# Rounding the mixed output weights in four pieces instead of two, in a fused attention and two-layer kernel

## The chip, the cores and the metric

The kernel runs on one core of one Trainium2 chip. The metric is the time of one execution on the device in microseconds (us), as the median of several runs. The core has five engines that run side by side and meet through semaphores: PE (matmuls, with its weight loads as PEld), DVE (VectorE), ACT (ScalarE), POOL (GpSimd) and SP, which here only issues DMAs.

## What is computed

```python
scores = scale * np.matmul(q, k.transpose(0, 1, 3, 2))        # 4 x 8 heads, 576 tokens, head size 64
thresh = np.max(scores, axis=-1, keepdims=True) - tau
scores = np.where(scores >= thresh, scores, -1000000000.0)
attn = softmax(scores)                                         # written out in the reference
x = np.matmul(attn, v)                                         # as 2304 x 512
h = x @ w_in                                                   # 512 x 2048
g = h * np.tanh(log1p(exp(h)))
x = g @ w_out                                                  # 2048 x 512
h = x @ w_in2
x = (h * np.clip(h + 3.0, 0.0, 6.0) / 6.0) @ w_out2
```

## The kernel before

The program has two stages. The first, some 330 us, is attention. The second, some 715 us, is the two layers, whose products are done by a scheme of seven products for eight (Strassen's, in Winograd's form), so each block of weights is needed as seven "mixes": sums and differences of its quarters. Each operand is split in a high part (the value rounded to the PE's fast 32-bit format, fp32r) and a low part (the rest), and three products of parts stand for one.

**Attention** walks over 32 heads in 8 turns (`it`) of 4 heads. A turn has 18 steps (`s`): two pairs of heads with 9 tiles of queries each, so steps 0 to 8 and 9 to 17 are two alike halves. In step `s`, by `attention_step` of each engine:

- PE makes the scores of tile t in two halves of 288 columns (L548), then spreads the sums in the third and fourth steps of a half (L581) or multiplies by the values (L601) in the other steps, then transposes tile t-2: first its tail of columns (L556), then the four main squares (L560). Before the second half of the scores it waits until ACT has kept the tail of tile t-2 (`after(pe, tail_kept, t - 2)`, with t that of the next step), and before the main squares until ACT has kept the main part of the tile before.
- ACT copies the transposed tail out of PSUM (`keep_tail`, L774), makes the exponentials of tile t (L793), and copies the transposed main part (`keep_main`, L758). In the third and fourth steps of a half a copy of the spread sums (L786) stands ahead of the tail. After steps 3 and 5 it rounds a head's keys (`round_k`, L745).
- DVE takes the maximum (L1010), weighs tile t-1 (L994), makes the threshold (L1021), and in steps 0 and 9 adds a small number to nine sums (`totals`, L1026) and inverts them. In steps 1, 6, 10 and 15 it scales an output (L1001); PE's spreading of sums waits for those of steps 1 and 10.
- POOL splits queries and keys of the coming heads (L1271 to L1283). In its order of one turn stand also, in this place: split of head 0, `mix_prep_in`, `mix_prep_out`, split of head 1, split of head 2, `rest_prep`, split of head 3. The split of head 2 ends with a wait for ACT's `round_k` of step 3.

**Preparation of the output weights.** A unit is one of 8 slices of one layer's output weights: 7 mixes of 256 columns on 128 partitions. It goes through `prep_out` (loaded by SP, mixed by POOL at L1300 or DVE at L1143), `prep_high` (rounded by ACT, `round_prep`, L806) and `prep_low` (`prep_out` less `prep_high`: `rest_prep`, POOL at L1306 for the first seven units, DVE at L1149 for the other nine), and SP stores both to DRAM (`store_prep_high`, `store_prep_low`). `PREP_PARTS` says in which pieces L806 and the subtractions are done:

```python
PREP_PARTS = (slice(0, 4), slice(4, MIXES))
...
if s == 16 and it < ITS - 1:
    round_prep(0, it, 0)
if s == 1 and it > 0:
    round_prep(0, it - 1, 1)
```

So seven units are rounded within the attention, one a turn: four mixes (1024 columns) after the `keep_main` of step 16, three (768 columns) after that of step 1 of the next turn. POOL's `rest_prep` of the unit comes after its wait for step 3. The other nine units are prepared in the layers (`late_unit`, `late_part`), in groups of products whose order on each engine is fixed in the code.

The order on every engine is that of the program; nothing reorders it. A wait holds all that stands behind it on its engine.

Of the kernel before, what the change touches and what calls it, by code (L numbers as in the profile page):

```python
# [14 lines left out]
def after(engine, semaphore, count):  # L15

    if isinstance(count, int) and count <= 0:
        return
    engine.wait_ge(semaphore, count)


def attention_and_layers(nc, qT, kT, v, tau, w_in1, w_out1, w_in2, w_out2, out):
# [16 lines left out]
    ITS = HEADS // HEADS_IT  # L39
# [13 lines left out]
    MIXES = 7  # L53
    A11_B11, S1_T1, S2_T2, S3_T3, A12_B21, S4_B22, A22_T4 = range(MIXES)
    QUADS = DFF // (2 * P)
# [96 lines left out]
    with ExitStack() as ctx:  # L152
# [3 lines left out]
        def sem(name):  # L156
            return ctx.enter_context(nc.semaphore(name))
# [51 lines left out]
        prep_out_rounded = sem("prep_out_rounded")  # L209
        prep_out_split = sem("prep_out_split")  # L210
# [37 lines left out]
        def f32(ap):  # L248
            return ap.bitcast(F32)

        def head_used(it, k):


            return it * TILES_IT + PAIR_TILES * (k // 2) + (MAIN + 1, PAIR_TILES)[k % 2]
# [47 lines left out]
        def late_unit(n):  # L302
            return divmod(QUADS - 1 + n, QUADS)


        def late_part(r, q):
            return divmod(GROUPS * r + q, 3) if r < SPANS else (LATE_UNITS, q)


        PREP_PARTS = (slice(0, 4), slice(4, MIXES))  # L310

        def g_slot(t, s):
            return t[:, s % G_RING, :]
# [47 lines left out]
        def _(sp):  # L361
# [44 lines left out]

            def store_prep_high(layer, u):

                sp.wait_ge(prep_out_rounded, 2 * (QUADS * layer + u) + 2)
                dst = w_out_mix[layer][:, u, :, :].rearrange("m p (h n) -> p m h n", h=2)  # L410
                sp.dma_start(dst[:, :, 0, :], f32(prep_high[:, :, :])).then_inc(prep_out_stored, 16)

            def store_prep_low(layer, u):

                sp.wait_ge(prep_out_split, 2 * (QUADS * layer + u) + 2)
                dst = w_out_mix[layer][:, u, :, :].rearrange("m p (h n) -> p m h n", h=2)
                sp.dma_start(dst[:, :, 1, :], f32(prep_low[:, :, :])).then_inc(prep_out_stored, 16)

# [49 lines left out]
            for r in range(ROUNDS):  # L468
                for q in range(QUADS):
                    unit, part = late_part(r, q)  # L470
# [265 lines left out]
        def _(act):  # L736
# [42 lines left out]
            def attention_step(it, s, ahead=True):  # L779

                t, p, i = it * TILES_IT + s, s // PAIR_TILES, s % PAIR_TILES
                first = isinstance(it, int) and it == 0
                if i in (2, 3) and (not first or p == 1):
                    u, pair = i - 2, it * PAIRS_IT + p - 1
                    act.wait_ge(spread_ready, 2 * pair + u + 1)
                    nc.scalar.copy(spread[:, PART_AT[u]:PART_AT[u + 1]], mixed[u]).then_inc(spread_kept, 1)  # L786
                if (not first or s >= 2) and (ahead or s < 2):
                    keep_tail(t - 2, (s - 2) % TILES_IT, it * PAIRS_IT + (s - 2) // PAIR_TILES)
                if ahead:
                    act.wait_ge(max_ready, t + 1)  # L790

                    after(act, probs_ready, t - 1)
                    nc.scalar.activation(halves(exps[:, s % 2, :]), scores[s % 3], ACT.Exp,  # L793
                                         bias=neg_max[:, s % 3:s % 3 + 1], scale=1.0).then_inc(exp_ready, 1)
                if (not first or s >= 2) and (ahead or s < 2):
                    keep_main(t - 2, (s - 2) % TILES_IT)
                if ahead and s in rounds:
                    round_k(it, rounds[s])

            def round_prep(layer, u, half):  # L800

                unit = QUADS * layer + u
                act.wait_ge(prep_out_mixed, 4 * unit + 4)
                after(act, prep_out_stored, 32 * unit)
                mixes = PREP_PARTS[half]
                nc.scalar.copy(prep_high[:, mixes, :], prep_out[:, mixes, :]).then_inc(prep_out_rounded, 1)  # L806

            def round_x(r, m):

                if m in X_MIXES:  # L810
                    act.wait_ge(x_mixed, 4 * r + X_MIXES.index(m) + 1)
                elif 0 < r < SPANS:
                    act.wait_ge(x_ready, 2 * PAIRS)
                elif r == 0:
                    act.wait_ge(x_ready, 4 * PAIRS_BATCH)
                else:
                    act.wait_ge(blocks_added, adds_before(r - SPANS + 1, 0))
                    act.wait_ge(c11_kept, r - SPANS + 1)
                after(act, slot_used, slots_before(r - 1, True))
                plain = {A11_B11: B11, A12_B21: B21, S4_B22: B22}  # L820
                src = x_block(r, plain[m]) if m in plain else x_mix[:, m, :, :]
                nc.scalar.copy(x_high[:, m, :, :], src).then_inc(x_high_ready, 1)
# [66 lines left out]
            for it in range(ITS):  # L889
                for s in range(TILES_IT):  # L890
                    attention_step(it, s)
                    if s == 16 and it < ITS - 1:
                        round_prep(0, it, 0)
                    if s == 1 and it > 0:
                        round_prep(0, it - 1, 1)
                    if it == ITS - 2 and s in (8, 10, 12):
                        round_x(0, X_ORDER[(8, 10, 12).index(s)])
                    if it == ITS - 1 and s in (2, 4, 6, 8):
                        round_x(0, X_ORDER[3 + (2, 4, 6, 8).index(s)])
                    if it == ITS - 1 and s == 16:  # L900
                        act.wait_ge(k_low_ready[HEADS_IT - 1], ITS)
                        act.wait_ge(scores_ready, head_used(ITS - 1, 1))
                        round_w(0, 0, 0)
                    if it == ITS - 1 and s == 17:
                        round_w(0, 0, 1)
# [15 lines left out]
            for r in range(ROUNDS):  # L921
                for q in range(QUADS):
                    if (r, q) == (0, 0):
                        continue
                    keep_first(r, q)
                    if q + 1 < QUADS:
                        round_w(r, q + 1, 0)
                    else:
                        for s in range(3):
                            round_g(r, s)  # L930
                    if q > 0:
                        gate(r, q - 1, B21)
                    if q + 1 < QUADS:
                        round_w(r, q + 1, 1)
                    else:
                        for s in range(3, G_RING):
                            round_g(r, s)
                    unit, part = late_part(r, q)
                    if unit < LATE_UNITS and part == 1:
                        for half in range(2):  # L940
                            round_prep(*late_unit(unit), half)
                    for b in (B22, B11, B12):
                        gate(r, q, b)
                gate(r, QUADS - 1, B21)
                for s in range(G_RING, SLOTS):
                    round_g(r, s)
                    if s == 13:
                        keep_first(r, QUADS)
                    if s == 45:
                        keep_c11(r)  # L950
                    if r + 1 < ROUNDS and s in ROUND_X_AT:
                        round_x(r + 1, X_ORDER[ROUND_X_AT.index(s)])
                if r + 1 < ROUNDS:
                    round_w(r + 1, 0, 0)
                    round_w(r + 1, 0, 1)
# [3 lines left out]
        def _(dve):  # L959
# [184 lines left out]

            def rest_prep(layer, u):

                for half, mixes in enumerate(PREP_PARTS):
                    dve.wait_ge(prep_out_rounded, 2 * (QUADS * layer + u) + half + 1)
                    nc.vector.tensor_tensor(prep_low[:, mixes, :], prep_out[:, mixes, :], f32(prep_high[:, mixes, :]),  # L1149
                                            ALU.subtract).then_inc(prep_out_split, 1)  # L1150

# [29 lines left out]
            for r in range(ROUNDS):  # L1181
                for q in range(QUADS):
# [16 lines left out]
                    unit, part = late_part(r, q)  # L1199
# [55 lines left out]
        def _(pool):  # L1255
# [45 lines left out]

            def rest_prep(u):

                for half, mixes in enumerate(PREP_PARTS):
                    pool.wait_ge(prep_out_rounded, 2 * u + half + 1)
                    nc.gpsimd.tensor_tensor(prep_low[:, mixes, :], prep_out[:, mixes, :], f32(prep_high[:, mixes, :]),  # L1306
                                            ALU.subtract).then_inc(prep_out_split, 1)

# [74 lines left out]
```

## Time and profile before

| | us |
|---|---|
| median of three runs | 1047.8 |
| lowest and highest | 1047.51, 1048.72 |
| the profiled execution | 1048.76 |
| its span, first to last instruction | 1046.6 |
| PE busy in the span | 1024.9 (98%) |
| DVE busy | 855.6 (82%) |
| ACT busy | 662.0 (63%) |
| POOL busy | 546.7 (52%) |

The profiled execution took 2.2 us more than its span and 1.0 us more than the median. PE is busy 98% of the span by this count, but a matmul counts as busy until its modelled end, and the next one is often issued before that: in attention the matmul row is full while the row of weight loads shows 5 to 6 tenths. Where the time goes there is seen in the distance between the same instruction of two steps. The granted clock of TensorE is 1.00 of full speed in all forty slices, its level of 2.4 GHz.

### The profile page before, as it was taken

Reading aid. Unit: us, or ns where it says so; the run is one execution under the profiler, and the core shown is the slowest. Engines: PE = TensorE matmul, PEld = TensorE weight load, DVE = VectorE, ACT = ScalarE, POOL = GpSimd, SP = SyncE. Lnnn points to the kernel's source line nnn. Section 1 sums busy time; section 2 is a strip of 40 time slices with the busy share of each in tenths; the row PEclk is TensorE's granted clock in tenths of the full one; section 3 lists DMA queues with packets and bytes.
Section 4 is the critical chain, followed back from the end, with each engine's and each line's share of the span. In section 5 each row is a group of like instructions: output and inputs, shape, how many; then the busy total and the mean of one; then the engine's idle time right before and its main releaser. Section 6 shows DMA issues by size and latency. Waiting matters only on the chain.

```text
span 1046.6 us, 19806 instructions
## 1 busy us (share of the span) xinstructions
PE 1024.9 (98%) x6856; PEld 920.5 (88%) x6856; DVE 855.6 (82%) x1694; ACT 662.0 (63%) x1241; POOL 546.7 (52%) x562
## 2 busy tenths in 40 slices
PE   6999999999999999999999999999999999999998
PEld 5666666666666999999999999999999999999998
DVE  7877877877773889978997889967996779968884
ACT  6778777778885566555664566646564655655643
POOL 7787887888983770078204770087103760068200
PEclk9999999999999999999999999999999999999999
DMA  6364564564542799869895899742785448843674
GB/s 189 103 215 144 161 215 143 162 215 140 177 146 82 225 327 308 321 199 294 297 371 187 266 328 315 289 142 106 250 310 163 165 164 274 281 151 127 221 242 161
DMA packets 136034, 224.37 MB, mean 214 GB/s; under 512 B 9216, under 2 KB 76288, under 8 KB 135936
## 3 DMA queue, kind: packets, MB, share of 16 engines
q1 hardware_dynamic: 135936, 223.12, 64.4%
q8 instruction: 55, 0.90, 0.3%
q14 instruction: 43, 0.35, 0.1%
HBM read 172.49 MB, written 50.59 MB: 213 GB/s over the span
## 4 chain that ended last, share of the span: by engine, by line
PE 79%; DVE 8%; ACT 7%; issue 4%; DMA 1%; SPq 0%; DVEq 0%; ACTq 0%
PE banks L601 8%; PE banks L548 7%; PE banks L666 7%; PE banks L668 7%; PE banks L667 7%; PE banks L703 6%; PE banks L702 6%; PE banks L701 6%; PE banks L709 5%; PE banks L711 5%; PE banks L710 5%; PE banks L560 5%; PE banks L556 3%; ACT relu L870 3%; PE banks L581 2%
## 5 line engine op out<-in xcount | busy, mean ns | idle before, releaser
L1330 POOL TENSOR_TENSOR ring<-raw,ring 128x256 fp32r<-128x256 f32 x336 | 282.3, 874 | 379.5 <-ACT ring L835 379.5
L666 PE MATMUL banks<-x_high,ring 128*128 128x384 f32 x672 | 226.7, 337 | 1.5 <-ACT probsT L774 0.8
L668 PE MATMUL banks<-x_high,ring 128*128 128x384 f32 x672 | 224.8, 334 | 0.0
L667 PE MATMUL banks<-x_low,ring 128*128 128x384 f32 x672 | 224.6, 334 | 0.0
L1010 DVE TENSOR_REDUCE neg_max<-banks 128x1 f32<-128x576 f32 x144 | 108.0, 750 | 55.6 <-PE banks L548 55.2
L703 PE MATMUL banks<-ring,g_low 128*128 128x256 f32 x504 | 142.6, 283 | 0.0
L702 PE MATMUL banks<-ring,g_high 128*128 128x256 f32 x504 | 142.6, 283 | 0.0
L701 PE MATMUL banks<-ring,g_high 128*128 128x256 f32 x504 | 142.6, 283 | 0.0
L666 PEld LDWEIGHTS banks<-x_high,ring 128*128 128x128 f32 x672 | 126.1, 188 | 7.7 <-issue 4.9
L667 PEld LDWEIGHTS banks<-x_low,ring 128*128 128x128 f32 x672 | 126.2, 188 | 0.0
L668 PEld LDWEIGHTS banks<-x_high,ring 128*128 128x128 f32 x672 | 126.1, 188 | 0.0
L885 ACT CAST g_high<-g_first 128x384 fp32r<-128x384 f32 x150 | 76.1, 513 | 67.0 <-PE banks L703 33.4
L548 PE MATMUL banks<-k_high,q_stack 128*128 128x288 f32 x320 | 105.1, 344 | 12.2 <-DVE k_low L985 7.7
L994 DVE SCALAR_TENSOR_TENSOR probs<-banks,thresh,exps 128x576 f32<-128x576 f32 x144 | 116.4, 808 | 0.7 <-ACT exps L793 0.7
L709 PE MATMUL banks<-g_high,ring 128*128 128x384 f32 x336 | 112.7, 335 | 0.3 <-DMA ring<-w_out_mix 0.3
L793 ACT ACTIVATE exps<-banks,neg_max 128x576 f32<-128x576 f32 x144 | 106.8, 742 | 9.5 <-DVE neg_max L1010 6.1
L711 PE MATMUL banks<-g_low,ring 128*128 128x384 f32 x336 | 112.3, 334 | 0.0
L710 PE MATMUL banks<-g_high,ring 128*128 128x384 f32 x336 | 112.3, 334 | 0.0
L601 PE MATMUL banks<-probsT,values 128*64 128x256 f32 (+3 forms) x640 | 103.9, 425 | 0.0
L703 PEld LDWEIGHTS banks<-ring,g_low 128*128 128x128 f32 x504 | 96.7, 192 | 0.0
L702 PEld LDWEIGHTS banks<-ring,g_high 128*128 128x128 f32 x504 | 96.7, 192 | 0.0
L701 PEld LDWEIGHTS banks<-ring,g_high 128*128 128x128 f32 x504 | 96.7, 192 | 0.0
(100 smaller groups left out, 2227.7 us busy)
## 6 DMA issues: line engine op xcount, KB each, us to landing
ring<-w_out_mix SPq DMA_DIRECT2D x168, 512.0 KB, 5.0
raw<-w_in_mix SPq DMA_DIRECT2D x48, 896.0 KB, 5.9
w_in_mix<-prep_in SPq DMA_DIRECT2D x18, 896.0 KB, 5.4
w_out_mix<-prep_high SPq DMA_DIRECT2D x16, 896.0 KB, 4.7
w_out_mix<-prep_low SPq DMA_DIRECT2D x16, 896.0 KB, 5.8
q_raw<-qT SPq DMA_DIRECT2D x64, 144.0 KB, 2.9
k_raw<-kT SPq DMA_DIRECT2D x64, 144.0 KB, 2.9
prep_in<-w_in SPq DMA_DIRECT2D x64, 128.0 KB, 3.3
```

What stands on the lines that cost most here:

```text
L548: mm = nc.tensor.matmul(scores[s % 3][:, half, :], lhs, rhs[:, HALF * half:HALF * (half + 1)], start=(n == 0), stop=(n == len(products) - 1))
L601: mm = nc.tensor.matmul(mixed[u][DH * a:DH * a + DH, :], values[rows, b, j, DH * a:DH * a + DH], probsT[b][rows, a, j, PART_AT[u]:PART_AT[ ...
L666: nc.tensor.matmul(dst, w[:, 0, cols], high, start=(t == 0 and m < 4), stop=False, skip_group_check=True)
L667: nc.tensor.matmul(dst, w[:, 0, cols], low, start=False, stop=False, skip_group_check=True)
L668: mm = nc.tensor.matmul(dst, w[:, 1, cols], high, start=False, stop=(t == KH - 1), skip_group_check=True)
L701: nc.tensor.matmul(to, high[:, rows], w[:, 0, :], start=begin and t % 2 == 0, stop=False, skip_group_check=True)
L702: nc.tensor.matmul(to, high[:, rows], w[:, 1, :], start=False, stop=False, skip_group_check=True)
L703: mm = nc.tensor.matmul(to, low[:, rows], w[:, 0, :], start=False, stop=end, skip_group_check=True)
L709: nc.tensor.matmul(dst[:, d, :], w[:, 0, cols], high, start=begin, stop=False, skip_group_check=True)
L710: nc.tensor.matmul(dst[:, d, :], w[:, 1, cols], high, start=False, stop=False, skip_group_check=True)
L711: mm = nc.tensor.matmul(dst[:, d, :], w[:, 0, cols], low, start=False, stop=end, skip_group_check=True)
L1330: nc.gpsimd.tensor_tensor(ring_slot(slot)[:, 1, :], raw[q % 2][:, m, :], f32(ring_slot(slot)[:, 0, :]), ALU.subtract).then_inc(w_low_ready, 1)
```

## The change

`PREP_PARTS` has four pieces, of 2, 2, 2 and 1 mixes (512, 512, 512 and 256 columns). In attention the first three are rounded after the `keep_main` of steps 15, 16 and 17, and the fourth after that of step 1. All places that walk over the pieces follow: the counts for which SP waits before it stores, and the subtractions on POOL and DVE, which become four each.

```diff
-        PREP_PARTS = (slice(0, 4), slice(4, MIXES))
+        PREP_PARTS = (slice(0, 2), slice(2, 4), slice(4, 6), slice(6, MIXES))
...
-                sp.wait_ge(prep_out_rounded, 2 * (QUADS * layer + u) + 2)
+                sp.wait_ge(prep_out_rounded, len(PREP_PARTS) * (QUADS * layer + u + 1))
...
-                sp.wait_ge(prep_out_split, 2 * (QUADS * layer + u) + 2)
+                sp.wait_ge(prep_out_split, len(PREP_PARTS) * (QUADS * layer + u + 1))
...
-            def round_prep(layer, u, half):
+            def round_prep(layer, u, n):
...
-                mixes = PREP_PARTS[half]
+                mixes = PREP_PARTS[n]
...
-                    if s == 16 and it < ITS - 1:
-                        round_prep(0, it, 0)
+                    if s in (15, 16, 17) and it < ITS - 1:
+                        round_prep(0, it, s - 15)
                     if s == 1 and it > 0:
-                        round_prep(0, it - 1, 1)
+                        round_prep(0, it - 1, 3)
...
-                        for half in range(2):
-                            round_prep(*late_unit(unit), half)
+                        for n in range(len(PREP_PARTS)):
+                            round_prep(*late_unit(unit), n)
...
-                for half, mixes in enumerate(PREP_PARTS):
-                    pool.wait_ge(prep_out_rounded, 2 * u + half + 1)
+                for n, mixes in enumerate(PREP_PARTS):
+                    pool.wait_ge(prep_out_rounded, len(PREP_PARTS) * u + n + 1)
```

DVE's `rest_prep` changes as POOL's does. PE and SP execute the same instructions in the same order as before.

First place: ACT at the end of a turn, from the main copy of step 15 on. Before:

```order
L758 COPY probsT_89<-banks 128x2x4x64
L774 COPY probsT_89<-banks 64x128
L793 ACTIVATE exps<-banks,neg_max 128x576
L758 COPY probsT_89<-banks 128x4x128
L806 CAST prep_high<-prep_out 128x1024
L774 COPY probsT_89<-banks 64x128
L793 ACTIVATE exps<-banks,neg_max 128x576
L758 COPY probsT_89<-banks 128x4x128
```

and in the change, the same steps 15 to 17:

```order
L758 COPY probsT_89<-banks 128x2x4x64
L806 CAST prep_high<-prep_out 128x512
L774 COPY probsT_89<-banks 64x128
L793 ACTIVATE exps<-banks,neg_max 128x576
L758 COPY probsT_89<-banks 128x4x128
L806 CAST prep_high<-prep_out 128x512
L774 COPY probsT_89<-banks 64x128
L793 ACTIVATE exps<-banks,neg_max 128x576
L758 COPY probsT_89<-banks 128x4x128
L806 CAST prep_high<-prep_out 128x512
```

One cast of 1024 columns has become three of 512, one after each of three steps.

Second place: ACT at step 1 of the next turn, with the copy of the spread sums of step 2 behind it. Before:

```order
L774 COPY probsT_89<-banks 64x128
L793 ACTIVATE exps<-banks,neg_max 128x576
L758 COPY probsT_89<-banks 128x4x128
L806 CAST prep_high<-prep_out 128x768
L786 COPY spread<-banks 128x256
L774 COPY probsT_80<-banks 64x128
```

and in the change:

```order
L774 COPY probsT_89<-banks 64x128
L793 ACTIVATE exps<-banks,neg_max 128x576
L758 COPY probsT_89<-banks 128x4x128
L806 CAST prep_high<-prep_out 128x256
L786 COPY spread<-banks 128x256
L774 COPY probsT_80<-banks 64x128
```

The cast at this place has shrunk from 768 columns to 256.

Third place: POOL, between the split of head 2 (its last line is the one that waits for `round_k` of step 3) and that of head 3. Before:

```order
L1283 TENSOR_TENSOR k_low_83<-k_raw_72,k_high_82 128x576
L1306 TENSOR_TENSOR prep_low<-prep_out,prep_high 128x1024
L1306 TENSOR_TENSOR prep_low<-prep_out,prep_high 128x768
L1271 TENSOR_TENSOR q_stack_84<-q_raw_71,q_scale 128x576
L1273 TENSOR_TENSOR q_raw_71<-q_raw_71,q_scale 64x576
```

and in the change:

```order
L1283 TENSOR_TENSOR k_low_83<-k_raw_72,k_high_82 128x576
L1306 TENSOR_TENSOR prep_low<-prep_out,prep_high 128x512 x3
L1306 TENSOR_TENSOR prep_low<-prep_out,prep_high 128x256
L1271 TENSOR_TENSOR q_stack_84<-q_raw_71,q_scale 128x576
L1273 TENSOR_TENSOR q_raw_71<-q_raw_71,q_scale 64x576
```

Two subtractions have become four over the same columns; all that follows on POOL stands behind them as before.

## Rows read from the trace of the kernel before

**Rows 1.** Busy time (count) of PE, PEld, DVE, ACT, POOL in most of layer one.

```profile
345.00:640.00 295.00, 294.57 (x1687) 291.53 (x1687) 265.48 (x434) 174.67 (x323) 132.60 (x151) 1.00 0.85 286
```

**Rows 2.** Casts and POOL's subtractions by tile: count, ns min/median/max, first and last start.

```profile
L806 ACT CAST prep_high<-prep_out x32: 829/945/1062, 42.3 to 626.6; 128x1024 fp32r<-128x1024 f32 x16, 128x768 fp32r<-128x768 f32 x16
...
L1306 POOL TENSOR_TENSOR prep_low<-prep_out,prep_high x14: 1827/2120/2398, 55.5 to 294.7; 128x1024 fp32r<-128x1024 f32 x7, 128x768 fp32r<-128x768 f32 x7
```

**Rows 3.** ACT in order of time (start, us) around one turn's casts, then step 8.

```profile
80.13 0.26 ACT L774 COPY probsT<-banks 64x128 f32<-64x128 f32 x1 [0.94 <-PE banks L556]
...
81.06 0.58 ACT L758 COPY probsT<-banks 128x512 f32<-128x512 f32 x1
81.52 1.06 ACT L806 CAST prep_high<-prep_out 128x1024 fp32r<-128x1024 f32 x1
82.61 0.26 ACT L774 COPY probsT<-banks 64x128 f32<-64x128 f32 x1
...
87.73 0.84 ACT L806 CAST prep_high<-prep_out 128x768 fp32r<-128x768 f32 x1
88.47 0.38 ACT L786 COPY spread<-banks 128x256 f32<-128x256 f32 x1
...
102.16 0.26 ACT L774 COPY probsT<-banks 64x128 f32<-64x128 f32 x1 [0.40 <-PE banks L556]
```

**Rows 4.** PE in order of time: transposes of steps 17, 2, 4; then 8, 11, 13.

```profile
81.67 0.33 PE L556 MATMUL banks<-ident,probs 128*128 128x128 f32 x1
...
82.92 0.40 PE L548 MATMUL banks<-k_high,q_stack 128*128 128x288 f32 x1 [0.23 <-ACT probsT L774]
...
87.79 0.33 PE L556 MATMUL banks<-ident,probs 128*128 128x128 f32 x1
...
89.19 0.40 PE L548 MATMUL banks<-k_high,q_stack 128*128 128x288 f32 x1 [0.37 <-ACT probsT L774]
...
92.83 0.33 PE L556 MATMUL banks<-ident,probs 128*128 128x128 f32 x1
...
101.80 0.33 PE L556 MATMUL banks<-ident,probs 128*128 128x128 f32 x1
...
102.66 0.30 PE L548 MATMUL banks<-k_high,q_stack 128*128 128x288 f32 x1
...
107.42 0.33 PE L556 MATMUL banks<-ident,probs 128*128 128x128 f32 x1
...
111.89 0.33 PE L556 MATMUL banks<-ident,probs 128*128 128x128 f32 x1
```

**Rows 5.** POOL in order of time: the mixing, later the subtractions of one unit.

```profile
74.56 3.16 POOL L1300 TENSOR_TENSOR prep_out<-prep_out 128x256 f32<-128x256 f32 x4
...
93.28 1.42 POOL L1283 TENSOR_TENSOR k_low<-k_raw,k_high 128x576 fp32r<-128x576 f32 x1 [5.20 <-ACT k_high L745]
94.65 4.16 POOL L1306 TENSOR_TENSOR prep_low<-prep_out,prep_high 128x1024 fp32r<-128x1024 f32 x2
```

**Rows 6.** DVE's totals and POOL beside them in order of time; ACT's wait behind.

```profile
84.22 1.14 POOL L1271 TENSOR_TENSOR q_stack<-q_raw,q_scale 128x576 fp32r<-128x576 f32 x1
85.03 0.37 DVE L1026 TENSOR_SCALAR totals<-sums 128x9 f32<-128x9 f32 x1
...
104.09 1.15 POOL L1271 TENSOR_TENSOR q_stack<-q_raw,q_scale 128x576 fp32r<-128x576 f32 x1
104.66 0.61 DVE L1026 TENSOR_SCALAR totals<-sums 128x9 f32<-128x9 f32 x1
...
163.40 0.86 DVE L1026 TENSOR_SCALAR totals<-sums 128x9 f32<-128x9 f32 x1
165.16 0.74 ACT L793 ACTIVATE exps<-banks,neg_max 128x576 f32<-128x576 f32 x1 [0.18 <-DVE neg_max L1010]
...
241.12 3.81 POOL L1317 TENSOR_TENSOR x_mix<-x 128x768 f32<-128x768 f32 x2
241.93 1.06 DVE L1026 TENSOR_SCALAR totals<-sums 128x9 f32<-128x9 f32 x1
```

More of the change, by code:

```diff
@@ L1145, in rest_prep @@
             def rest_prep(layer, u):
-                for half, mixes in enumerate(PREP_PARTS):
-                    dve.wait_ge(prep_out_rounded, 2 * (QUADS * layer + u) + half + 1)
+                for n, mixes in enumerate(PREP_PARTS):
+                    dve.wait_ge(prep_out_rounded, len(PREP_PARTS) * (QUADS * layer + u) + n + 1)
                     nc.vector.tensor_tensor(prep_low[:, mixes, :], prep_out[:, mixes, :], f32(prep_high[:, mixes, :]),
@@ L1302, in rest_prep @@
             def rest_prep(u):
-                for half, mixes in enumerate(PREP_PARTS):
-                    pool.wait_ge(prep_out_rounded, 2 * u + half + 1)
+                for n, mixes in enumerate(PREP_PARTS):
+                    pool.wait_ge(prep_out_rounded, len(PREP_PARTS) * u + n + 1)
                     nc.gpsimd.tensor_tensor(prep_low[:, mixes, :], prep_out[:, mixes, :], f32(prep_high[:, mixes, :]),
```

## The prediction

> **What bounds the kernel now.** I read first where PE has room. In the layers it has none: weight loads alone fill 291.5 of 295 us [rows 1], so nothing that ACT, DVE or POOL does there moves the end unless it stalls PE. Attention is another matter. There I read the order in time of PE and measured from one transpose L556 to the same one some steps on. A turn has two alike halves, and only one holds the casts of the weights, so the other is the control. From step 17 to step 2 of the next turn PE takes 87.79 - 81.67 = 6.12 us, from step 8 to step 11 it takes 107.42 - 101.80 = 5.62. From step 2 to 4 it takes 92.83 - 87.79 = 5.04, from 11 to 13 it takes 111.89 - 107.42 = 4.47 [rows 4]. So a turn loses 0.50 and 0.57 us, and in each of the two stretches PE's second half of the scores stands at a wait for ACT's copy of the tail (0.23 and 0.37 us idle, the rest being overlap lost) [rows 4]. The wait ends late because the copy stands behind a cast: 1.06 us after step 16, 0.84 us after step 1 [rows 3]. Seven units are rounded in attention, so the two places hold 7 x 1.07 = 7.5 us of the span.
>
> **ACT's part of the change.** Cast prices: (1.06 - 0.84) / 256 = 0.86 ns a column with 0.18 us fixed [rows 3], so 512 columns take 0.62 us and 256 take 0.40. A unit pays for two more instructions, 2 x 0.18 = 0.36 us of ACT, but ACT has 0.40 us idle ahead of a tail copy in an undisturbed step [rows 3], and what counts is how late each tail comes.
> - Step 15: ahead of the tail at 80.13 ACT idles 0.94 us [rows 3]; a cast of 0.62 hides.
> - Step 16: from the main copy to the next tail 82.61 - 81.06 = 1.55 us with 1024 columns [rows 3], so 1.55 - 0.44 = 1.11 with 512. The tail then starts at 82.17, 0.50 after its L556 at 81.67. In the undisturbed step 8 it starts 102.16 - 101.80 = 0.36 after. PE was released 82.92 - 82.61 = 0.31 after the tail's start [rows 3, 4], which gives 0.81; undisturbed, the first matmul of the second half starts 102.66 - 101.80 = 0.86 after L556 [rows 4]. Cost 0, at most 0.05; 0.03 taken, since all behind the tail is 0.14 late too.
> - Step 17: the main copy is 0.14 late from the cast before, another 1.11 puts the next tail 0.6 after its L556, 0.24 later than undisturbed, of which PE can take 0.19 less 0.05 to be safe (0.31 + 0.36 is 0.67 against 0.86). Cost 0.09, between 0 and 0.24.
> - Step 1: the cast with the spread copy behind it shrinks from 0.74 us [rows 3] to 0.74 - 0.44 = 0.30. Of the 0.57 lost there 0.44 goes and 0.13 stays (between 0 and 0.2).
>
> So 0.25 of the 1.07 us stays: 7 x 0.82 = 5.7 us gained, with 4.5 and 7 as ends.
>
> **POOL's and DVE's part.** POOL's subtraction costs (2.398 - 1.827) / 256 = 2.2 ns a column with 0.11 us fixed [rows 2]; from the k_low row of 576 columns (1.42) [rows 5] the fixed part is nearer 0.20. Two more instructions, each overlapping its neighbour by 0.05 (93.28 to 94.65 is 1.37 for a row of 1.42) [rows 5], put all behind them on POOL 0.26 us later; ends 0.1 and 0.4. POOL itself has time: it idles 5.2 us ahead of the k_low of step 3 [rows 5], and that wait pins its phase to ACT once a turn. The price comes by another way. DVE's L1026 on nine columns takes 0.37, 0.61, 0.86 or 1.06 us, and it always ends when the POOL instruction then running does: 85.03 + 0.37 = 85.40 against 84.22 + 1.14 = 85.36; 104.66 + 0.61 = 105.27 against 104.09 + 1.15 = 105.24; 241.93 + 1.06 = 242.99 against half of 3.81 after 241.12, 243.03 [rows 6]. It is held by POOL. Up to 0.61 that harms nobody; at 0.86 ACT's exponentials of step 1 wait 0.18 us for DVE [rows 6], so the room is used up at 0.68 for ACT, a little later for PE (0.71 taken), and what is above comes out one for one.
> - Step 9: POOL 0.26 later makes 0.61 into 0.87, cost 0.16 us. Seven turns: 1.2 us (the last, with other work on POOL, taken at 0.25).
> - Step 0: POOL is 0.26 later while DVE comes 0.50 - 0.16 = 0.34 earlier against it. L1026 began 0.81 after POOL's L1271 [rows 6]; now 0.81 - 0.60 = 0.21 after it, and lasts 1.15 + 0.02 - 0.21 = 0.96, cost 0.25. Four turns of that kind: 1.0. In the turn of the row at 241.93 POOL's instruction is 1.9 us long, so 1.06 becomes 1.9 + 0.02 - 0.21 = 1.7: 1.0 against 0.35 paid now, 0.65 more. In the turn of the row at 163.40 POOL had come late, and DVE now lands in the instruction before: 0.15 is saved. The seventh changes little. Sum 1.5.
> Where PE is already 0.1 late from ACT, DVE's lateness counts for less, which takes 0.4 off: 1.2 + 1.5 - 0.4 = 2.3 us given back. Ends: 0, and 4.5 with every L1026 held to POOL's next end.
>
> A rule of the Trainium skill bears on this: the page "GPSIMD Engine Reference", section "8. Key points", says that POOL shares its interfaces to SBUF with DVE and contends with DVE instructions in a two-port mode or with two SBUF inputs. The rows agree for L1026, and show more than contention, since the short instruction waits for the long one's end. By the rule alone one could not say which way the phase moves; that is read from the rows.
>
> Against the change speaks the page "VectorE: DVE Perf Modes", section "The TRN2 errata", by which each ScalarE instruction with an SBUF source pays 224 cycles, an estimated 0.19 us at 1.2 GHz; 14 more casts would be 2.6 us if none were hidden. The 0.18 us fixed read above agrees, and the idle time ahead of the tails speaks for hiding most of it.
>
> **The layers.** Nine units: ACT 18 more casts, 0.18 each, 0.36 a unit beside PE; DVE 18 more subtractions. Their fixed part has no row of its own; POOL's 0.20 for the same instruction bounds it, so 0.4 a unit at most. PE lacks 0.4 us in 295 [rows 1], its inputs being ready well ahead. Cost 0, ends -0.3 (DVE may start on a smaller first piece) and 1. SP stores when four pieces are counted, 0.3 us later; its loads for the next unit come as much later as POOL wants them later. 0.
>
> **Sum.** 5.7 - 2.3 = 3.4 us less. The profiled execution of 1048.8 would be 1045.4; the median lies 1.0 below it: 1047.8 - 3.4 = 1044.4 us.
>
> **Rivals.**
> 1. *Casts hide, and the lock costs nothing.* DVE could slip in ahead of POOL's instruction in step 0: its margin is the 0.21 us above. Then the sum is the 5.7 alone: 1042.1. For it: the margin is small, and one unforeseen shift of either engine decides. Against: the margin is a difference in which POOL's lag falls out, as step 9 passes it on to DVE.
> 2. *The lock takes most of the gain.* If POOL falls 0.4 us behind or more, both L1026 of a turn are held 1.1 us and up, 0.4 each: 4.5 given back, and 1.2 gained: 1046.6, no change that can be told. Against: POOL's fixed part read from two pairs of rows.
> 3. *Slower: the cast of step 15 waits for the mixing.* Before, the first cast came a step later. Mixing ends at 74.56 + 3.16 = 77.72 [rows 5]. The cast does no harm if it is done by the tail at 80.13 [rows 3], so if it starts by 79.5: room 1.8 us, 1.5 after POOL's lag. Beyond that tail, exponentials and main copy all stand behind it, and PE loses what it is late, less the 0.2 it can take. The 3.4 us are outweighed from 3.4 / 7 + 0.2 = 0.7 us beyond the room, a lag of POOL or of a load of 2.5 us in every turn; at 3 us of lag it would be 7 x 0.5 = 3.5 slower than before: 1051.3. No row shows POOL nearly that late.
>
> **How the numbers follow.** The limit between a change and none is 0.2%, 2.1 us, about what a measurement of this kernel can tell: faster is below 1045.7. Chances: the forecast 0.55, of which nearly all is below that; rival 1, 0.20; rival 2, 0.20; rival 3 and other slower ones, 0.05. That gives faster 0.75, same 0.20, slower 0.05. The range reaches to rival 1 and nearly to rival 2: 1042.0 to 1046.4.
>
> **What would show it.** PE from L556 of step 17 to that of step 2: 5.62 plus 0.1 from ACT plus what L1026 adds; from 2 to 4: 4.6. Waits of PE for the tail (L774) down from 0.6 us a turn to some 0.2. L1026 at 0.87 in step 9 and 0.96 in step 0. POOL's four subtractions 0.26 us longer from first start to the next split. Attention 3.4 us shorter, layers the same. I am wrong if the tail waits stay, if L1026 does not follow POOL's ends, or if the layers change by over 1 us.

## The result, and the profile after

The changed kernel takes 1050.5 us (median of 7 runs, 1050.3 to 1052.7), the kernel before in the same comparison 1047.6 (7 runs). The ratio is 1.0033, 95% interval 1.0021 to 1.0044: slower by 2.9 us, where 3.4 us less had been forecast, and outside the range. The sign is wrong, and the two traces say at once which half of the argument was: attention came out nearly as worked out, the layers did not. The traced execution of the changed kernel is the slowest of its seven, 2.2 us above their median, and that of before some 1 us above its own, so the two traces lie 4.0 us apart where the medians lie 2.9.

In attention, PE's transposes of the same steps as in [rows 4], steps 17, 2 and 4, then 8, 11 and 13, from the timeline of the changed kernel:

```profile
81.42 0.33 PE L556 MATMUL banks<-ident,probs 128*128 128x128 f32 x1
...
87.40 0.33 PE L556 MATMUL banks<-ident,probs 128*128 128x128 f32 x1
...
92.03 0.33 PE L556 MATMUL banks<-ident,probs 128*128 128x128 f32 x1
...
101.00 0.33 PE L556 MATMUL banks<-ident,probs 128*128 128x128 f32 x1
...
106.82 0.33 PE L556 MATMUL banks<-ident,probs 128*128 128x128 f32 x1
...
111.23 0.33 PE L556 MATMUL banks<-ident,probs 128*128 128x128 f32 x1
```

| PE's transposes, us | before | forecast | after |
|---|---|---|---|
| step 17 to 2 | 6.12 | 5.97 | 5.98 |
| step 2 to 4 | 5.04 | 4.60 | 4.63 |
| step 8 to 11 | 5.62 | 5.78 | 5.82 |
| step 11 to 13 | 4.47 | 4.47 | 4.41 |

(The forecast of 17 to 2 is 5.62 and 0.10 for ACT's lateness and 0.25 for L1026. Over the turns this stretch takes 5.82 to 5.98 us, and 6.67 in the turn with POOL's long instruction; the other three repeat within 0.03 in most turns.) From the transpose of step 0 in the second turn to that after the last turn, the changed kernel takes 276.1 us against 278.8: 2.7 us less, from seven turns.

The totals L1026 and the POOL instruction beside them, in order of time, which answer to [rows 6]:

```profile
84.17 1.15 POOL L1271 TENSOR_TENSOR q_stack<-q_raw,q_scale 128x576 fp32r<-128x576 f32 x1
84.35 1.00 DVE L1026 TENSOR_SCALAR totals<-sums 128x9 f32<-128x9 f32 x1
...
103.60 1.15 POOL L1271 TENSOR_TENSOR q_stack<-q_raw,q_scale 128x576 fp32r<-128x576 f32 x1
103.86 0.92 DVE L1026 TENSOR_SCALAR totals<-sums 128x9 f32<-128x9 f32 x1
```

L1026 starts 0.18 us after POOL's instruction in step 0 and lasts 1.00; in step 9 it lasts 0.92. Both end when POOL's does (85.35 against 85.32, 104.78 against 104.75), as in [rows 6], and near the 0.96 and 0.87 of the forecast.

In the layers I look first at the windows of 295 us as in [rows 1]: PE, PEld, DVE, ACT and POOL with their counts, of the changed kernel.

```profile
345.00:640.00 295.00, 292.71 (x1653) 284.71 (x1651) 266.93 (x442) 173.58 (x333) 127.79 (x148) 1.00 0.84 281
```

The column to read is PEld: 284.7 us of weight loads against 291.5 before, 36 loads fewer in the same time. The loads fill 6.8 us less. A stretch around one late unit, in the timelines, shows where PE waits. Before (DVE's `add_u` L1061 once a quad of products, the subtractions L1149, the adds L1082, ACT's gate L872 and its copy L847):

```profile
365.99 0.56 DVE L1061 TENSOR_TENSOR middle<-banks,first_kept 128x384 f32<-128x384 f32 x1 [0.36 <-ACT first_kept L847]
...
368.98 2.68 DVE L1149 TENSOR_TENSOR prep_low<-prep_out,prep_high 128x1024 fp32r<-128x1024 f32 x2 [0.41 <-ACT prep_high L806]
371.58 1.21 DVE L1082 TENSOR_TENSOR g_first<-banks,middle 128x384 f32<-128x384 f32 x2
372.16 0.53 ACT L872 ACTIVATE g_first<-g_first 128x384 f32<-128x384 f32 x1 [1.69 <-DVE g_first L1082]
372.59 0.46 ACT L847 COPY first_kept<-banks 128x384 f32<-128x384 f32 x1
373.14 0.56 DVE L1061 TENSOR_TENSOR middle<-banks,first_kept 128x384 f32<-128x384 f32 x1 [0.35 <-ACT first_kept L847]
```

and the changed kernel, the same instructions:

```profile
363.02 0.56 DVE L1061 TENSOR_TENSOR middle<-banks,first_kept 128x384 f32<-128x384 f32 x1 [0.35 <-ACT first_kept L847]
...
365.57 4.35 DVE L1149 TENSOR_TENSOR prep_low<-prep_out,prep_high 128x512 fp32r<-128x512 f32 x4
369.85 1.21 DVE L1082 TENSOR_TENSOR g_first<-banks,middle 128x384 f32<-128x384 f32 x2
370.43 0.53 ACT L872 ACTIVATE g_first<-g_first 128x384 f32<-128x384 f32 x1 [2.74 <-DVE g_first L1082]
370.86 0.46 ACT L847 COPY first_kept<-banks 128x384 f32<-128x384 f32 x1
371.41 0.56 DVE L1061 TENSOR_TENSOR middle<-banks,first_kept 128x384 f32<-128x384 f32 x1 [0.35 <-ACT first_kept L847]
371.43 0.19 PEld L666 LDWEIGHTS banks<-x_high,ring 128*128 128x128 f32 x1 [0.88 <-POOL ring L1330]
...
372.75 0.19 PEld L666 LDWEIGHTS banks<-x_high,ring 128*128 128x128 f32 x1 [0.31 <-issue]
```

DVE subtracts the same 1792 columns in 4.35 us instead of 2.68. It starts without the wait of 0.41 for ACT, so some 1.25 us of lateness are left. Behind it stands the add L1082, for which ACT's gate waits; behind the gate on ACT stands the copy L847 of the next quad, and for that copy PE's fifth product of the quad waits (`first_copied`). PE's weight loads stand still for 0.88 us, and for 0.31 more at 372.75, where the sixth product follows DVE's add L1070. The quad takes 371.41 - 363.02 = 8.39 us instead of 7.15. The profile names POOL as the releaser of PE, but POOL's last instruction had ended at 370.53; the last to end before PE went on was L847, at 371.32. Following L1061 through both traces, the changed kernel is 2.97 us ahead when the layers begin, falls back by 1.2 us in five quads, all of them behind a unit's subtractions with POOL busy, and is 4.03 us behind at the end: 7.0 us lost in the layers, 6.1 of them in those five. POOL is busy beside six of the nine units. The first, at 345.5 us in the trace of before, lost nothing in the end; in the three beside which POOL idles the subtractions take 2.23 us instead of 2.08, and no quad falls back. The unit shown above is one of three such. In the other two of the five DVE starts without a wait for ACT in both kernels, and takes 1.22 us more; one of them, before and after:

```profile
463.77 3.17 DVE L1149 TENSOR_TENSOR prep_low<-prep_out,prep_high 128x1024 fp32r<-128x1024 f32 x2
```
```profile
461.48 4.39 DVE L1149 TENSOR_TENSOR prep_low<-prep_out,prep_high 128x512 fp32r<-128x512 f32 x4
```

### The profile page after: what moved, and what is told of

The parts are those of the page before. It is cut to its first block, busy times and chain, and to the rows that moved or that the text cites. A ratio compares the mean times of both kernels' runs of the same rounds, so it can differ in the third digit from the quotient of the medians.

```text
span 1050.6 us, 19900 instructions
## 1 busy us (share of the span) xinstructions
PE 1029.3 (98%) x6856; PEld 920.7 (88%) x6856; DVE 867.2 (83%) x1712; ACT 665.0 (63%) x1273; POOL 547.6 (52%) x576
## 4 chain that ended last, share of the span: by engine, by line
PE 74%; DVE 12%; ACT 6%; issue 5%; DMA 3%; SPq 0%; DVEq 0%; ACTq 0%
PE banks L601 9%; PE banks L548 8%; PE banks L703 6%; PE banks L702 6%; PE banks L701 6%; PE banks L560 6%; PE banks L666 5%; PE banks L709 5%; PE banks L711 5%; PE banks L710 5%; PE banks L668 5%; PE banks L667 5%; PE banks L556 3%; ACT relu L870 3%; DMA ring<-w_out_mix 2%
```

## The experiments

All variants but e8 are of the changed kernel, with the pieces given apart for the seven early units and the nine late ones. REST stands for the subtractions (POOL early, DVE late), ROUND for ACT's casts; a piece of subtraction waits for the casts that cover it. Theory A is the price of DVE's instructions beside POOL's, theory B that ACT's four casts delay its gates.

**e1_late_two**, the late units back in two pieces:

```diff
+        ROUND_EARLY = (slice(0, 2), slice(2, 4), slice(4, 6), slice(6, MIXES))
+        ROUND_LATE = (slice(0, 4), slice(4, MIXES))
+        REST_EARLY = (slice(0, 2), slice(2, 4), slice(4, 6), slice(6, MIXES))
+        REST_LATE = (slice(0, 4), slice(4, MIXES))
```

> Attention as in the change (casts of 2, 2, 2, 1 mixes, four subtractions on POOL), the nine units of the layers as before (casts and subtractions of 4 and 3 mixes). Theory A (in the layers each subtraction of DVE waits for the POOL instruction then running, so four pieces take 4.35 us where two took 2.68, and DVE is what PE waits for there): the layers fall back to their old time, attention keeps its 3.0 us: 1044.6 us. Theory B (ACT's four casts in the layers delay the gates) gives the same here. Theory C (the layers lose by something that comes from attention ending earlier, as the phase of the engines or DMAs): it stays near 1050.

Measured: 1044.3 us against 1048.0 of before in that comparison, ratio 0.9965 (0.9952 to 0.9977). The gain of attention stands by itself once the layers are left alone, so theory C of the expectation, a loss that comes from attention ending earlier, falls. A and B are not told apart by this run.

**e2_late_act_four** and **e3_late_dve_four** part ACT's casts from DVE's subtractions:

```diff
# e2, against e1
-        ROUND_LATE = (slice(0, 4), slice(4, MIXES))
+        ROUND_LATE = (slice(0, 2), slice(2, 4), slice(4, 6), slice(6, MIXES))
# e3, against e1
-        REST_LATE = (slice(0, 4), slice(4, MIXES))
+        REST_LATE = (slice(0, 2), slice(2, 4), slice(4, 6), slice(6, MIXES))
```

> As e1_late_two, but ACT makes four casts a unit in the layers too; DVE subtracts in two pieces. Theory A: as e1_late_two within 0.5 us, 1044.6 to 1045.1, since ACT waits for DVE there anyway. Theory B: near the changed kernel, 1050.

> As e1_late_two, but DVE subtracts in four pieces in the layers; ACT makes two casts. Theory A: near the changed kernel, 1050.5, with four subtractions taking some 4.3 us beside POOL. Theory B: 1044.6.

Measured: e2 1045.2 us, 0.9975 (0.9964 to 0.9986); e3 1052.0 us, 1.004 (1.0025 to 1.0055). By its ratio e3 lies 0.7 us above the changed kernel, and the intervals overlap. The same window of the layers of e1, e2 and e3, in this order:

```profile
345.00:640.00 295.00, 294.74 (x1690) 292.06 (x1689) 265.52 (x440) 175.66 (x324) 129.25 (x148) 1.00 0.86 288
```
```profile
345.00:640.00 295.00, 294.92 (x1692) 292.49 (x1691) 265.65 (x441) 177.11 (x340) 129.54 (x148) 1.00 0.87 288
```
```profile
345.00:640.00 295.00, 292.90 (x1657) 285.51 (x1657) 266.26 (x446) 173.11 (x319) 127.20 (x147) 1.00 0.84 281
```

Sixteen more casts of ACT in the window (x324 to x340) leave PE's loads at 292.5 us; DVE's pieces alone take them to 285.5. Theory B falls, and the loss is DVE's. It is not DVE's own fixed cost either: with POOL idle two more pieces cost 0.15 us (2.08 and 2.23), with POOL busy 1.22 (3.17 in e1 and 4.39 in e3, the same unit). Of these, 0.15 are DVE's own and some 0.54 a piece are the wait for POOL.

**e8_before_late_four**, the kernel before with the pieces of the layers alone:

```diff
+        ROUND_EARLY = (slice(0, 4), slice(4, MIXES))
+        ROUND_LATE = (slice(0, 2), slice(2, 4), slice(4, 6), slice(6, MIXES))
+        REST_EARLY = (slice(0, 4), slice(4, MIXES))
+        REST_LATE = (slice(0, 2), slice(2, 4), slice(4, 6), slice(6, MIXES))
```

> The kernel before with only its layers changed: casts and subtractions of the nine late units in four pieces, attention as it was. If attention and layers are two independent terms, it loses what the layers lost in the changed kernel, 7.0 us: 1054.6 to 1055. If the loss needs attention to end earlier: near 1047.8.

Measured: 1055.4 us against 1048.5, ratio 1.0066 (1.005 to 1.0083), 7.0 us slower. Loss and gain add up as independent terms: 7.0 from the layers here less 3.8 gained in e1 is 3.2, and the change lost 2.9.

**e7_late_dve_seven** doubles the suspected cost once more:

```diff
# against e1
-        REST_LATE = (slice(0, 4), slice(4, MIXES))
+        REST_LATE = tuple(slice(m, m + 1) for m in range(MIXES))
```

> As e3_late_dve_four, but DVE subtracts in seven pieces of one mix in the layers. Theory A, with a price for each instruction (each waits for one POOL instruction, 1.17 us a piece): 7 x 1.17 = 8.2 us instead of 4.35 where POOL is busy, 3.8 us more in each of five to six units, so 19 to 23 us over e3_late_dve_four: near 1071. If the price goes by columns (two engines sharing bandwidth), it doesn't change: near 1052.

Measured: 1053.9 us, 1.0049 (1.0034 to 1.0064). That is 1.9 over e3 (1.5 when each is taken against before in its own comparison), where I had expected some 19. There is a price by the instruction, but it is 0.96 us for a piece of 256 columns and not 1.17, and it has a cap that I had not seen. Single instructions, by narrow windows of a line's own view (count, ns, start): DVE's pieces of 1024 columns (before), of 512 (changed) and of 256 (e7), all with POOL busy.

```profile
L1149 DVE TENSOR_TENSOR prep_low<-prep_out,prep_high x1: 1761/1761/1761, 463.8 to 463.8; 128x1024 fp32r<-128x1024 f32 x1
```
```profile
L1149 DVE TENSOR_TENSOR prep_low<-prep_out,prep_high x1: 1178/1178/1178, 365.6 to 365.6; 128x512 fp32r<-128x512 f32 x1
```
```profile
L1166 DVE TENSOR_TENSOR prep_low<-prep_out,prep_high x2: 953/956/958, 364.5 to 365.4; 128x256 fp32r<-128x256 f32 x2
```

and POOL's 256-column subtractions beside two of them, in the changed kernel and in e7:

```profile
L1330 POOL TENSOR_TENSOR ring<-raw,ring x2: 1061/1122/1183, 365.1 to 366.2; 128x256 fp32r<-128x256 f32 x2
```
```profile
L1347 POOL TENSOR_TENSOR ring<-raw,ring x2: 917/920/924, 364.3 to 365.2; 128x256 fp32r<-128x256 f32 x2
```

While both engines have such instructions they take turns: 1.18 us for a DVE piece of 512 and 1.18 for the POOL instruction beside it, 0.96 and 0.92 with 256. Starts in the traces lie 1.15 and 0.88 us apart on both engines. Without POOL four pieces take 2.23 us and seven 2.43. With it the three kinds of unit take, in e3, 3.86, 3.90 and 4.39 us, and in e7 4.05, 4.66 and 4.60. So a piece pays some 0.54 us, one turn of POOL, and 0.07 of its own, for as long as POOL has an instruction left, and POOL had three, five and four of its seven of that quad left or running when DVE came. Where it had three or four, four pieces had already met them all, and seven cost 0.2 us more, their own fixed cost; where it had five, seven met one more, and cost 0.76 more. There, in e7, the first piece took 0.47 us, four took 0.96, and the last two, with POOL out of work, 0.41. The rows of that unit: e3 in the timeline, then e7, the group and the whole in the timeline.

```profile
364.66 3.90 DVE L1166 TENSOR_TENSOR prep_low<-prep_out,prep_high 128x512 fp32r<-128x512 f32 x4 [0.42 <-ACT prep_high L823]
```
```profile
L1166 DVE TENSOR_TENSOR prep_low<-prep_out,prep_high x7: 414/953/959, 364.1 to 368.4; 128x256 fp32r<-128x256 f32 x7
```
```profile
364.15 4.66 DVE L1166 TENSOR_TENSOR prep_low<-prep_out,prep_high 128x256 fp32r<-128x256 f32 x7 [0.41 <-ACT prep_high L823]
```

**e4_pool_two** gives POOL back its two pieces in attention:

```diff
# against e1
-        REST_EARLY = (slice(0, 2), slice(2, 4), slice(4, 6), slice(6, MIXES))
+        REST_EARLY = (slice(0, 4), slice(4, MIXES))
```

> As e1_late_two, but POOL subtracts in two pieces in attention, so it does not lag by 0.26 us a turn; ACT's casts stay four. If DVE's L1026 is held to the end of POOL's running instruction, it is back at 0.61 in step 9 and 0.80 in step 0, which gives back 0.15 us in step 11 and 0.1 in step 2 of most turns, 1.2 to 1.7 in all: 1043 to 1043.4. If POOL's pieces don't matter: 1044.6, as e1_late_two.

Measured: 1043.6 us, 0.996 (0.9944 to 0.9976); e1 and e4 can't be told apart by their medians (0.7 us), but the traces show the mechanism, and there the seven turns take 274.5 us against 276.0, 1.5 less, where 1.2 to 1.7 was expected. L1026 has become L1043 here:

```profile
82.81 0.79 DVE L1043 TENSOR_SCALAR totals<-sums 128x9 f32<-128x9 f32 x1
...
102.15 0.59 DVE L1043 TENSOR_SCALAR totals<-sums 128x9 f32<-128x9 f32 x1
```

0.79 in step 0 and 0.59 in step 9, as expected, and the transposes of steps 10 to 11 are 1.81 us apart again where e1 has 1.97 to 2.01.

**e5_casts_421** takes away what is left of ACT's lateness, **e6_no_totals** the instruction that POOL holds:

```diff
# e5, against e4
-        ROUND_EARLY = (slice(0, 2), slice(2, 4), slice(4, 6), slice(6, MIXES))
+        ROUND_EARLY = (slice(0, 4), slice(4, 6), slice(6, MIXES))
...
-                    if s == 1 and it > 0:
-                        round_prep(0, it - 1, 3)
# e6, against e5
-                    nc.vector.tensor_scalar(totals[:, b, :], sums[:, b, :], 1e-9, None, ALU.add).then_inc(totals_ready, 1)
-                    dve.wait_ge(totals_ready, pair + 1)
-                    nc.vector.reciprocal(recips[:, b, :], totals[:, b, :]).then_inc(recips_ready, 1)
+                    nc.vector.reciprocal(recips[:, b, :], sums[:, b, :]).then_inc(recips_ready, 1)
```

> As e4_pool_two, but ACT rounds a unit of attention in pieces of 4, 2 and 1 mixes after steps 15, 16 and 17, and nothing after step 1: the largest cast (1.06 us) stands where ACT idles 0.94 us, and the copy of the spread sums has no cast ahead. If what is left at PE is ACT's lateness (0.21 us in steps 0 and 1, 0.15 in step 3), 7 x 0.36 = 2.5 us go; DVE comes 0.07 us earlier against POOL, so L1026 of step 0 grows to 0.87 and up to 1 us comes back: 1041.1 to 1042.1. If those steps are long for another reason: 1043.6, as e4_pool_two.

> As e5_casts_421, with DVE's addition of 1e-9 to the sums (L1026) left out; the reciprocal reads the sums. The addition is work of nine columns, 0.17 us when it waits for nobody. If its wait for POOL is what costs PE (0.1 to 0.15 us in most steps 2, 0.9 in one turn, 0.4 in the last step 11), the whole goes: 2 us less than e5_casts_421, near 1039.5. If the reciprocal takes over the wait, or the lateness was harmless: the same as e5_casts_421.

Measured: e5 1041.3 us, 0.9934 (0.9919 to 0.9948), as expected; e6 1040.3 us, 0.9921 (0.9906 to 0.9936). PE's transposes in e6 (L573), steps 17, 2, 4, then 8, 11, 13:

```profile
80.74 0.33 PE L573 MATMUL banks<-ident,probs 128*128 128x128 f32 x1
...
86.45 0.33 PE L573 MATMUL banks<-ident,probs 128*128 128x128 f32 x1
...
90.92 0.33 PE L573 MATMUL banks<-ident,probs 128*128 128x128 f32 x1
...
99.89 0.33 PE L573 MATMUL banks<-ident,probs 128*128 128x128 f32 x1
...
105.51 0.33 PE L573 MATMUL banks<-ident,probs 128*128 128x128 f32 x1
...
109.99 0.33 PE L573 MATMUL banks<-ident,probs 128*128 128x128 f32 x1
```

Step 17 to 2 takes 5.71 and 2 to 4 takes 4.47, against 5.62 and 4.48 in the half that never had a cast. Of the 1.07 us a turn only 0.08 is left. In e5 the totals were held for 0.82 us in step 0 and 1.62 in the turn in which POOL's instruction is 1.8 us long; in e6 the reciprocal stands in their place and takes 0.20 us beside a busy POOL:

```profile
83.33 1.15 POOL L1284 TENSOR_TENSOR q_stack<-q_raw,q_scale 128x576 fp32r<-128x576 f32 x1
...
83.69 0.20 DVE L1041 RECIPROCAL recips<-sums 128x9 f32<-128x9 f32 x1
```

The gain of e6 over e5 was expected at 2 us and came out at 1.0, which the scatter of the runs (1 us) does not separate from 2; in the traces the seven turns take 271.6 us against 273.1, 1.5 less.

**e9_late_one** and **e10_best_again**, in one comparison:

```diff
# e9, against e6
-        ROUND_LATE = (slice(0, 4), slice(4, MIXES))
+        ROUND_LATE = (slice(0, MIXES),)
-        REST_LATE = (slice(0, 4), slice(4, MIXES))
+        REST_LATE = (slice(0, MIXES),)
```

> As e6_no_totals, but each of the nine late units is one cast on ACT and one subtraction on DVE. By the alternation of DVE and POOL each DVE instruction fewer saves some 0.65 us of DVE where POOL is busy; but in the version with two pieces PE is already without a stall there (0.4 us in 295), so theory A gives no change at PE: within 0.5 us of e10_best_again. If the rest stall of the layers came from these units, up to 1 us less.

> The same kernel as e6_no_totals once more, for a tighter interval: 1039.5 to 1041, a ratio of 0.992 to the kernel before.

Measured: e9 1040.6 us, 0.9925 (0.9912 to 0.9937); e10, the kernel of e6 again, 1040.8 us, 0.9925 (0.9911 to 0.9938). The one piece takes 2.02 to 2.13 us in eight units and 2.56 in the first, and PE's loads had hardly a stall left that it could remove (2.7 us of idle time in the 295 us in e6, 2.9 in e9), so fewer pieces than two bring nothing. The kernels of e6 and e9 can't be told apart and are the fastest that were run, some 7 us faster than before and 10 faster than the change. Both leave out the addition of 1e-9 to sums that are at least 1, since each row's largest term is exp(0).

## Why the prediction was wrong, point by point

- **What bounds the kernel:** half right. Attention was read rightly, by the alike halves of a turn. Of the layers I read [rows 1], that PE's loads fill 291.5 of 295 us, and concluded that nothing else moves the end "unless it stalls PE", and then that its inputs were "ready well ahead". They were not. DVE was busy 265 of those 295 us by the same row, and the rows of before in the section on the result show its subtractions ahead of the chain L1082, L872, L847 to PE. The quad shown took 7.15 us before and 8.39 after, that behind the unit at 463.8 us 7.86 and 9.07. Most other quads there are 7.58 us apart by L1061, before and after alike, with DVE working almost without a break, while the 42 weight loads of a quad take 7.3 us at 0.1735 each: DVE's chain was no faster than PE even before.
- **ACT's part:** right in mechanism, a little short in size. 0.25 us a turn was to stay of 1.07. In e4, where L1026 is nearly harmless, steps 17 to 2 take 5.82 and 2 to 4 take 4.62 in most turns, so 0.20 and 0.14 stay, 0.34 in all.
- **POOL's and DVE's part in attention:** right in mechanism and near in size. POOL's subtractions took 4.46 us instead of 4.16, 0.30 more for 0.26 forecast, L1026 0.92 and 1.00. Some luck is in this: the row of 1.42 us gives 0.15 us fixed and not 0.20 (576 columns at 2.2 ns are 1.27). In the turn with POOL's long instruction L1026 took 1.70, the 1.7 of the forecast. Rival 1 (DVE slips in ahead) came true in one of the four turns of that kind, where L1026 took 0.27 us. Rival 2 had POOL 0.4 us late or more, and POOL was 0.30 late; what came back is an estimated 2.4 us (7.5, less 7 x 0.34, less the 2.7 gained), for 2.3 forecast.
- **The layers: the step that failed.** The sentence was: "Their fixed part has no row of its own; POOL's 0.20 for the same instruction bounds it, so 0.4 a unit at most", and from it "Cost 0, ends -0.3 and 1". I priced a DVE instruction alone, though shortly before I had shown that POOL holds DVE. Alone the price is even less than I allowed, 0.15 us a unit. Where POOL is busy two more pieces make DVE 1.2 us later in all five units that count (3.17 to 4.39 in two; 2.68 to 4.35 less the wait of 0.41 in three): 1.2 us in each of five quads, 6.1 of the 7.0 us. Rows of before held it: the subtractions in pairs took 2.08 us in three units, 2.68 and 3.17 in the others, with the same columns, and four DVE instructions of 256 columns with SBUF inputs took 1.80 us at 340.21 (L1143), where POOL idled, and 3.59 at 353.34 (L1134), where it worked. A spread of durations in one group of like instructions was the sign, and I did not follow it.
- **The page "GPSIMD Engine Reference"** of the Trainium skill names, in its section "8. Key points", two kinds of DVE instruction that contend with POOL: those in a two-port mode and those with two SBUF inputs. I used the first kind alone. L1149 reads `prep_out` and `prep_high`, two SBUF inputs, and is the second kind. The traces agree: a piece of 512 columns takes 0.69 us with POOL idle and up to 1.22 beside it, and DVE's adds L1061, L1070 and L1082, which have one input in PSUM, take 0.54 to 0.56 us for 384 columns whether POOL runs or not. By that rule, read to its end, the layers should have been a rival with a price.
- **Rival 3**, slower, had the wrong place: the cast of step 15 did not wait for the mixing in any turn, steps 15 to 16 being 2.44 to 2.45 us before and after.
- **Sum:** -3.4 forecast; by the traces -3.0 at the start of the layers and +7.0 in them, which is 4.0 us slower; by the medians 2.9 slower. The 3.4 stands for attention alone, and e1, with the layers as before, gained 3.8.

What stays open: the other 0.9 of the 7.0 us is the sum of small steps both ways, of 0.6 us at most, outside the five quads. In the trace of e8 the five quads take 6.1 us again while the layers as a whole take 5.8, so these small steps differ from trace to trace. No run took them apart.

## What to carry to other kernels

Cutting work in pieces is priced by the instruction, and the price is not the engine's own fixed cost alone: ask what runs beside it on an engine with which it must take turns. Pieces pay off where they fit idle time (ACT in attention) and cost where the engine's instructions stand in line with another's (DVE beside POOL), so the two stages of one kernel want different pieces. When like instructions of like size differ in duration by a third, find out why before pricing one more of them.

## What the runs showed of the hardware that was not expected

- DVE's subtractions with both inputs in SBUF and POOL's alternate one by one, and both are slowed: 1024 columns take 1.22 us alone (the unit at 395 us) and 1.76 beside POOL, 512 take 0.69 and 1.22, 256 take 0.42 and 0.96, and POOL's 256-column subtraction takes 0.74 alone and up to 1.7 beside a DVE piece of 1024 columns. In every unit of e3 and e7 beside which POOL works the number of encounters is the smaller of DVE's pieces and the instructions that POOL has left, which is why seven pieces cost DVE but 0.2 us more than four in most units, and 0.76 in those where POOL has five left.
- A DVE addition on nine columns from SBUF to SBUF is held until POOL's running instruction ends: in all 32 cases of the two traces it ends 0.03 us after it, at the soonest after 0.17 us and at the latest after 1.70. A reciprocal on the same nine columns at the same place is not held (0.20 to 0.21 us in all 16 cases of e6, POOL busy).
- Attention was predicted to 0.06 us a stretch, in the turn worked out, from differences of 0.1 us in start times. Where the rows of one engine repeat to 0.02 us from turn to turn, such working is sound; what fails is what it leaves out.
